# The passage from attention to the first expert layer: where the first expert is counted, when the exponential runs, and where the turned w2 lies

## The chip, the cores and the metric

One core of a Trainium2 chip runs one program. The metric is the device time of one execution in microseconds (us), as the median of several runs. A second number comes from one profiled execution: its span from the first to the last instruction, with every instruction's start and length.

## The reference

```python
scores = scale * np.matmul(z, z.transpose(0, 2, 1))       # 4 batches of 2496 rows, d_qk 64
x = u * np.matmul(np.maximum(scores, 0.0) ** 2, v)        # 9984 rows of 256
# first expert layer, 8 experts, hidden width 1024
do_compute = x @ w_skip > 0
e_idx = argmax(x @ w_gate); gate_w = softmax of the chosen expert
y = gate_w * (relu(x @ w1[e]) @ w2[e]);  x = x + y where do_compute
# second expert layer: logits = x @ w_gate2 + modality_bias[modality_id], the same form, all rows
```

Products are taken in fp32 split into a high and a low part (H and L in the names), three matmuls for one.

## The kernel before

Attention is worked off in 20 chunks of 512 tokens. In each chunk TensorE (PE) makes scores (L1406) and the sums with v (L1417), ScalarE (ACT) takes relu and square, VectorE (DVE) splits the result into AH and AL. One chunk behind, each chunk's 512 rows are routed: PE makes the logits (`route`, L1476) and turns the rows (L1465 in `transpose_x`), DVE picks the experts (`pick_experts`, L1003 to L1019), ACT takes the exponential (`exp_chunk`, L662) and copies the rows (`xrow_half`, L658), PE counts the ranks (`prefixes`, L1488), DVE sets gates (`set_gates`, L1032) and addresses (`place_rows`, L1048 to L1052), and GpSimd (POOL) scatters the rows into `token_rows` in HBM, one indirect DMA for each 128 rows (`scatter_chunk`, L522). Each group of rows (expert of layer one, or of layer two for rows that skip layer one) has its own stretch of `token_rows`, and `base` counts them.

After the last chunk there is no attention work left beside the routing; this stretch is called the passage below. Each engine has its own queue and does its instructions in the order in which its block is written; they meet at semaphores.

- PE: 48 filling matmuls (`keep_warm`), `route`, 6 fillers, `route_rows`, 34 fillers, `prefixes`, `gate_columns(0)` (L1535), `transpose_in` of the first tile (L1553), 16 fillers, the wait for `cum_ready`, then for each expert `gate_parts` (L1545), `gate_columns` of the next expert, and the expert's tiles of 256 rows.
- DVE: sums and product with u, `row_meta` (L991, waits for the scatter of the chunk before), counting of the first expert (`plan_first`), `pick_experts`, `set_gates`, `place_rows`, `finish_groups` (the tile bounds `cum`, last instruction L1187, which sets `cum_ready`), `xt_low`, `plan_second`, a wait for the last scatter, the low part of the gate columns (L1279), the tiles.
- ACT: `sums`, `xrow_half` 0 and 1, `copy_gcols(0)` (L747), `exp_chunk`, the first tile's copies (L777, L778), the wait for `cum_ready`, then for each expert `gpart_split_high` and `copy_gcols` of the next.
- POOL: scatter of chunk 19, `load_w2t(0)` (L483, 1 MB), a wait for `gate_columns(0)`, `load_w2t(1)` into the same place, scatter of chunk 20 (L522; numbers count routed chunks from 1).
- SP: waits for `early_ready` (from `plan_first`) and for the scatter of chunk 19, then loads the first expert's full tiles (L378).

Gate columns are w2 of an expert times the second layer's gate weights; with them the tile's own second product also gives the next layer's logits. `gate_columns(e)` needs w2 of expert e with its axes turned (`w2t_raw`), and lies in the buffer A, which is attention's.

A tile of layer one is 24 matmuls (`layer1(0)`, L1604), four turns, 24 matmuls (`layer1(2)`) and 48 of `layer2` (L1621). The first `layer2` needs the first low part from DVE (`h_low(0)`, L1285). Before its first tile DVE waits on all scattered rows:

```python
xt_low(0, 0)
plan_second()
dve.wait_ge(rows_stored, 64 * (CHUNKS + 1))
```

Of the kernel before, what the change touches and what calls it, by code (L numbers as in the profile page):

```python
# [15 lines left out]
P = 128  # L16
# [44 lines left out]
def bass_attention_two_moe(nc, u, v, z, w_skip, w_gate, w1, w2, modality, w_gate2, bias2, w2t, out):  # L61
    xs = nc.dram_tensor("token_rows", (GR * CAP + SPARE, ROW), F32, kind="Internal").ap()

    with ExitStack() as ctx:
# [6 lines left out]
        def sem(name):  # L71
            return ctx.enter_context(nc.semaphore(name))
# [50 lines left out]
        R = [sb(f"R{i}", [P, QW]) for i in range(2)]  # L123
        A_all = sb("A", [P, NA * QW])
        A = [A_all[:, i * QW:(i + 1) * QW] for i in range(NA)]
        w2t_raw = A_all[:, 0:KD * F].rearrange("p (k f) -> p k f", k=KD)
# [108 lines left out]
        w2t_loaded = sem("w2t_loaded")  # L235
# [208 lines left out]
        def _(pool):  # L444
# [36 lines left out]
            def load_w2t(e):  # L481

                pool.dma_start(w2t_raw, w2t[e, :, :].rearrange("(k p) f -> p k f", p=P)).then_inc(w2t_loaded, 16)  # L483
# [85 lines left out]
            scatter_chunk(CHUNKS - 1)  # L569
            wait(al_ready, 2 + KT * CHUNKS)  # L570
            load_w2t(0)
            wait(gcols_made, 1)
# [10 lines left out]
            for ph in range(2):  # L583
# [14 lines left out]
                for at in range(E):  # L598
# [3 lines left out]
                    def ahead():  # L602
                        if ph == 0:
                            if at + 2 < E:
                                wait(gcols_made, at + 2)
                                load_w2t(at + 2)
                            next_weights(turn_, at % 2, False)
                        else:
                            with pool.If(hi < total):
                                next_weights(turn_, at % 2, True)  # L610
# [26 lines left out]
        def _(act):  # L637
# [120 lines left out]
            xrow_half(CHUNKS, 0)  # L758
            xrow_half(CHUNKS, 1)
            copy_gcols(0)  # L760
            exp_chunk(CHUNKS)

            for ph in range(1):
# [14 lines left out]
                s_.copy(xkeep[:, 0:1, :, :].rearrange("p o s d -> p (o s d)"), xin[:, :, :].rearrange("p s d -> p (s d)")).then_inc(q.x_kept, 1)  # L778
                act.wait_ge(cum_ready, ph + 1)
# [15 lines left out]
                for at in range(E):  # L795
                    hi = end_of(act, ph, at)
                    turn_, h = at + ph * E, at % 2
                    if ph == 0:
                        gpart_split_high(at)
                        if at + 1 < E:  # L800
                            copy_gcols(at + 1)
# [130 lines left out]
        def _(dve):  # L932
# [145 lines left out]
            V_AT = {0: (1,), 1: (2, 3), 2: (4,), 5: (5, 6), 6: (7,), 7: (8,), 8: (9,)}  # L1078
            z_low(0)
# [27 lines left out]
            final_done = [0]  # L1107

            def f(ins):

                final_done[0] += 1
                ins.then_inc(final_step, 1)
                dve.wait_ge(final_step, final_done[0])

            def by_turn(out_, in_):
                f(v_.tensor_tensor(pair[:, 0:E, :], perm[:, :, :], in_[:, None, :].to_broadcast([P, E, E]), ALU.mult))
                f(v_.tensor_reduce(out_, pair[:, 0:E, :], AX.X, ALU.add))

            def full_first(ph, rows):

                f(v_.tensor_scalar(early_f[:, ph:ph + 1], rows, float(TILE[ph]), None, ALU.is_ge))
                f(v_.tensor_scalar(two_f[:, :], rows, float(2 * TILE[ph]), None, ALU.is_ge))
                f(v_.tensor_tensor(early_f[:, ph:ph + 1], early_f[:, ph:ph + 1], two_f[:, :], ALU.add))
                v_.tensor_copy(early[:, ph:ph + 1], early_f[:, ph:ph + 1]).then_inc(early_ready, 1)

# [21 lines left out]
            def plan_first(ph):  # L1150

                full_first(ph, cnt[:, 0:1])

            dve.wait_ge(u_loaded, 16 * CHUNKS)
            for d in range(KD):
                sum_rows(CHUNKS, d).then_inc(o_summed, 1)
                dve.wait_ge(o_summed, 2 * CHUNKS + 1 + d)
                v_.tensor_tensor(xT[:, d, :], xT[:, d, :], uT[:, d, :], ALU.mult).then_inc(x_ready, 1)
            row_meta(CHUNKS)

            dve.wait_ge(base_ready, CHUNKS)
            f(v_.tensor_tensor(cnt[:, :], base[:, :], group0[:, :], ALU.subtract))
            plan_first(0)
            pick_experts(CHUNKS)
# [39 lines left out]
            for ph in range(1):  # L1204
# [61 lines left out]

                xt_low(0, 0)
                if ph == 0:
                    plan_second()
                    dve.wait_ge(rows_stored, 64 * (CHUNKS + 1))  # L1270
                lo = 0
                for at in range(E):
                    hi = end_of(dve, ph, at)
                    turn_ = at + ph * E
                    if ph == 0:
                        dve.wait_ge(gpart_high, at + 1)
                        for s in range(2):
                            part, wh, wl = gate_part(s, at % 2)
                            ins = v_.tensor_tensor(wl, part, wh.bitcast(F32), ALU.subtract)  # L1279
                        ins.then_inc(gpart_low, 1)  # L1280
# [102 lines left out]
        def _(pe):  # L1383
# [142 lines left out]
            def gate_columns(e):  # L1526

                pe.wait_ge(w2t_loaded, 16 * e + 16)
                if e > 0:
                    pe.wait_ge(gcols_copied, e)  # L1530
                for q in range(2):
                    for kd in range(KD):
                        for j in range(QT):
                            f = q * QT + j
                            last = t_.matmul(pO[CG * j:CG * j + CG, 2 * QW + q * P:2 * QW + (q + 1) * P], wg[:, kd, :], w2t_raw[:, kd, f * P:(f + 1) * P],  # L1535
                                             start=(kd == 0), stop=(kd == KD - 1), skip_group_check=True)
# [19 lines left out]
            keep_warm(pS[0], 48)  # L1556
# [3 lines left out]
            keep_warm(pS[0], 34)  # L1560
            prefixes(CHUNKS)
            gate_columns(0)
            pe.wait_ge(xrow_copied, 2 * CHUNKS + 2)

            for ph in range(1):
# [3 lines left out]
                keep_warm(pS[0], 16)  # L1569
# [10 lines left out]
                for at in range(E):  # L1580
                    hi = end_of(pe, ph, at)
                    h = at % 2
                    if ph == 0:
# [177 lines left out]
```

## Time and profile before

| what | us |
|---|---|
| median of 3 runs (lowest to highest) | 1518.81 (1516.99 to 1521.19) |
| the profiled execution's own time | 1520.95 |
| its span | 1519.4 |
| PE busy | 1480.8 (97%) |
| DVE, ACT, POOL busy | 1010.5, 772.6, 398.6 |
| the last attention matmul starts | 725.7 |
| the first expert matmul starts | 744.23 |

Times in rows are from the span's start. A row of a timeline is a run of like instructions on one engine; in brackets stands how long the engine had been idle and who released it. A name such as `pO<-A,wg` is the tile written and those read. The granted clock is PE's, as a share of 2.4 GHz. The end of a matmul is modelled, so starts are the safer reading.

### The profile page before, as it was taken

The page shows a single profiled execution, that of the slowest core. Times are in us where ns is not written, and L with a number is a line of the kernel's source. Part 1 is how long each engine was busy: PE and PEld are TensorE (multiplying, and loading weights), DVE is VectorE, ACT ScalarE, POOL GpSimd, SP SyncE. Part 2 cuts the span into 40 slices and gives each one's busy share as a digit, 9 for nine tenths or more (in the row PEclk, how much of TensorE's full clock was granted, in tenths as well). Part 3 has the DMA queues.
Part 4 walks back from the last instruction along what each step waited for, and adds up shares of the span by engine and source line. Part 5 has one row for each costly group of instructions (what it writes and reads, how often), then busy time and mean ns, then how long its engine had stood idle before and what let it go on. Part 6 is the DMA issues. An engine that isn't in the chain of part 4 may idle for free.

```text
span 1519.4 us, 34233 instructions
## 1 busy us (share of the span) xinstructions
PE 1480.8 (97%) x11713; PEld 1285.9 (85%) x11713; DVE 1010.5 (67%) x2377; ACT 772.6 (51%) x1504; POOL 398.6 (26%) x371
## 2 busy tenths in 40 slices
PE   8999999999999999999899999999999999999995
PEld 7887888788887888788799999998888888888884
DVE  7989987999779998977566666665333433333331
ACT  6676766776666767666344444444332333333331
POOL 4133312334223433311222232224221221211211
PEclk9999999999999999999999999999999999999998
DMA  5302030202312020200433363322211121111110
GB/s 118 98 30 64 28 99 28 65 30 58 90 32 68 28 83 30 85 30 28 162 101 132 131 217 131 105 95 83 86 54 43 42 68 45 42 50 50 42 47 24
DMA packets 57888, 107.83 MB, mean 71 GB/s; under 512 B 17879, under 2 KB 32226, under 8 KB 57756
## 3 DMA queue, kind: packets, MB, share of 16 engines
q0 software_dynamic: 18336, 58.68, 11.0%
q1 hardware_dynamic: 39420, 47.48, 11.0%
q8 instruction: 72, 1.18, 0.3%
q14 instruction: 60, 0.49, 0.1%
HBM read 75.63 MB, written 32.04 MB: 71 GB/s over the span
## 4 chain that ended last, share of the span: by engine, by line
PE 85%; DVE 5%; issue 4%; DMA 3%; POOL 1%; ACT 1%; SPq 0%; POOLq 0%; ACTq 0%; DVEq 0%
PE pO L1417 26%; PE pS L1661 11%; PE pO L1673 10%; PE pS L1621 9%; PE pO L1604 9%; PE pS L1406 7%; PE pO L1675 5%; PE pM L1661 3%; DVE AH L1073 2%; DMA raw<-in_v_dram 2%; PE pT L1652 1%; PE pT L1465 1%; DMA token_rows<-xrow,dest 1%; DVE AL L1075 1%; PE pT L1553 1%
## 5 line engine op out<-in xcount | busy, mean ns | idle before, releaser
L1075 DVE TENSOR_TENSOR AL<-A,AH 128x512 fp32r<-128x512 f32 (+1 forms) x400 | 318.4, 796 | 13.7
L1417 PE MATMUL pO<-AH,VH 64*128 64x512 f32 (+1 forms) x1520 | 299.5, 384 | 6.6 <-DVE xT L983 4.8
L1417 PE MATMUL pO<-AL,VH 64*128 64x512 f32 (+1 forms) x1520 | 298.0, 382 | 0.0
L1417 PE MATMUL pO<-AH,VL 64*128 64x512 f32 (+1 forms) x1520 | 297.8, 381 | 0.0
L695 ACT ACTIVATE R<-pS 128x512 f32<-128x512 f32 (+1 forms) x400 | 213.7, 588 | 149.5 <-PE pS L1406 141.1
L1073 DVE CAST AH<-A 128x512 fp32r<-128x512 f32 (+1 forms) x400 | 222.7, 557 | 42.4 <-ACT A L704 41.8
L704 ACT ACTIVATE A<-R 128x512 f32<-128x512 f32 (+1 forms) x400 | 228.8, 624 | 15.9 <-DVE AL L1075 15.7
L1673 PE MATMUL pO<-VL,AH 128*128 128x512 f32 x640 | 232.4, 399 | 0.0
L1332 DVE SCALAR_TENSOR_TENSOR AL<-pS,AH 128x512 fp32r<-128x512 f32 x120 | 83.0, 692 | 180.1 <-ACT AH L861 179.3
L1675 PE MATMUL pO<-VL,AL 128*128 128x256 f32 x640 | 179.5, 280 | 0.0
L1417 PEld LDWEIGHTS pO<-AH,VH 64*128 64x128 f32 x1520 | 147.8, 184 | 33.6 <-issue 9.2
L580 POOL DMA_INDIRECT out_dram<-xrow,tok_at x80 | 77.9, 974 | 368.2 <-DVE xrow L1342 349.9
L861 ACT ACTIVATE AH<-pS 128x512 fp32r<-128x512 f32 x120 | 71.8, 599 | 195.2 <-PE pS L1661 193.0
L1417 PEld LDWEIGHTS pO<-AL,VH 64*128 64x128 f32 x1520 | 147.8, 184 | 23.0
L1417 PEld LDWEIGHTS pO<-AH,VL 64*128 64x128 f32 x1520 | 147.9, 184 | 22.4
L1661 PE MATMUL pS<-ZH,VH 128*128 (+1 forms) x480 | 165.1, 391 | 0.7 <-issue 0.4
L1673 PEld LDWEIGHTS pO<-VL,AH 128*128 128x128 f32 x640 | 120.2, 188 | 25.6
L1604 PE MATMUL pO<-ZH,VH 128*128 x736 | 129.6, 289 | 0.0
L541 POOL TENSOR_TENSOR xT<-xT,uT 128x512 f32<-128x512 f32 x38 | 50.5, 1340 | 300.6 <-DVE xT L983 300.6
L1675 PEld LDWEIGHTS pO<-VL,AL 128*128 128x128 f32 x640 | 120.6, 188 | 3.2
L1621 PE MATMUL pS<-VL,AH 128*128 128x264 f32 x736 | 120.7, 286 | 0.0
L522 POOL DMA_INDIRECT token_rows<-xrow,dest x80 | 85.9, 1074 | 101.0 <-issue 99.8
(232 smaller groups left out, 2412.3 us busy)
## 6 DMA issues: line engine op xcount, KB each, us to landing
raw<-in_w_dram POOLq DMA_DIRECT2D x22, 1024.0 KB
A<-token_rows SPq DMA_DIRECT2D x21, 536.0 KB
uT<-in_u_dram SPq DMA_DIRECT2D x16, 512.0 KB
A<-in_w2t_dram POOLq DMA_DIRECT2D x8, 1024.0 KB
xin<-token_rows SPq DMA_DIRECT2D x24, 268.0 KB
raw<-in_v_dram SPq DMA_DIRECT2D x4, 1152.0 KB, 6.0
raw<-in_v_dram SPq DMA_DIRECT2D x4, 768.0 KB, 7.7
raw<-in_z_dram SPq DMA_DIRECT2D x8, 368.0 KB
```

Of the source, the lines that this page charges most:

```text
L522: g_.indirect_dma_start(xs, bass.IndirectOffsetOnAxis(dest[:, j:j + 1], 0), xrow[:, j, :], None, bounds_check=GR * CAP - 1, oob_is_err=Fal ...
L695: s_.activation(R[k % 2][:, 0:n], pS[k % 2][:, 0:n], ACT.Relu, scale=1.0 / S).then_inc(relu_done, 1)
L704: s_.activation(A[k % NA][:, 0:n], R[k % 2][:, 0:n], ACT.Square).then_inc(square_done, 1)
L1073: v_.tensor_copy(AH[k % NBUF][:, 0:n], A[k % NA][:, 0:n]).then_inc(ah_ready, 1)
L1075: v_.tensor_tensor(AL[k % NBUF][:, 0:n], A[k % NA][:, 0:n], AH[k % NBUF][:, 0:n].bitcast(F32), ALU.subtract).then_inc(al_ready, 1)
L1406: last = t_.matmul(pS[r][:, 0:n], w[rows, (2 * p + r) * P:(2 * p + r + 1) * P], x[rows, zc:zc + n], start=(m == 0), stop=(m == 2))
L1417: last = t_.matmul(pO[:, (KD * r + d) * QW:(KD * r + d) * QW + n], vv[rows, vo + k * D + d * P:vo + k * D + (d + 1) * P], a[k % NBUF][rows ...
L1604: last = t_.matmul(pO[:, bank * 512 + fi * TT:bank * 512 + (fi + 1) * TT], w[h][:, kd, f * P:(f + 1) * P], x[:, ds(par, 1), kd, :].rearran ...
L1621: last = t_.matmul(pS[s][:, 0:width], a[p][:, fi * TT + s * P:fi * TT + (s + 1) * P], w[h][:, f, 0:width], start=(f == 0 and n == 0), stop ...
L1661: last = t_.matmul(ring[f % RING][:, :], w[h][:, kd, f * P:(f + 1) * P], x[:, ds(par, 1), kd, :].rearrange("p o t -> p (o t)"), start=(n = ...
L1673: t_.matmul(pO[:, s * QW:(s + 1) * QW].rearrange("p (m d) -> p m d", m=2), AH[f][:, rows], w2hl[h][:, :, f, 0:D], start=(f == 0), stop=(f ...
L1675: last = t_.matmul(pO[:, s * QW:s * QW + D], AL[f][:, rows], w2h[h][:, f, 0:D], start=False, stop=(f == NF - 1), skip_group_check=True)
```

## The change

- DVE counts the first expert (`plan_first`) inside the last attention chunk, after `place_rows(19)`. After the sums it goes straight to `pick_experts`; `row_meta` comes behind that.
- ACT takes the exponential between the two halves of `xrow_half`. `gpart_split_high(0)` and `copy_gcols(1)` come ahead of the wait for `cum_ready`.
- The turned w2 has two places: A for even experts, and for odd ones the unused end of `raw` together with R (two buffers made one). Each load is two DMAs of 512 KB. `load_w2t(0)` comes ahead of the scatter of chunk 19, `load_w2t(1)` behind it and behind the last attention matmul; later loads wait for one `gate_columns` less.
- DVE makes the low part of expert 0's gate columns ahead of `plan_second` and of the wait for the scattered rows.
- PE: 40 fillers ahead of `route` in place of 48; `gate_columns(0)` and 6 fillers ahead of `prefixes` in place of 34 fillers; `gate_parts(0)`, `gate_columns(1)` and 40 fillers ahead of the wait for `cum_ready`, in place of 16 fillers there and of the two gate steps behind it.

```diff
-        R = [sb(f"R{i}", [P, QW]) for i in range(2)]
+        R_all = sb("R", [P, 2 * QW])
+        R = [R_all[:, i * QW:(i + 1) * QW] for i in range(2)]
-        w2t_raw = A_all[:, 0:KD * F].rearrange("p (k f) -> p k f", k=KD)
+        w2t_raw = [[A_all[:, 0:F], A_all[:, F:2 * F]], [raw[:, 2 * KD * F:(2 * KD + 1) * F], R_all[:, :]]]
...
@@ POOL
-                pool.dma_start(w2t_raw, w2t[e, :, :].rearrange("(k p) f -> p k f", p=P)).then_inc(w2t_loaded, 16)
+                for kd in range(KD):
+                    pool.dma_start(w2t_raw[e % 2][kd], w2t[e, kd * P:(kd + 1) * P, :]).then_inc(w2t_loaded[e % 2], 16)
...
-            scatter_chunk(CHUNKS - 1)
             wait(al_ready, 2 + KT * CHUNKS)
             load_w2t(0)
-            wait(gcols_made, 1)
+            scatter_chunk(CHUNKS - 1)
+            wait(pv_done, NBUF + KT * CHUNKS)
             load_w2t(1)
             scatter_chunk(CHUNKS)
...
-                                wait(gcols_made, at + 2)
+                                wait(gcols_made, at + 1)
                                 load_w2t(at + 2)
@@ ACT
             xrow_half(CHUNKS, 0)
+            exp_chunk(CHUNKS)
             xrow_half(CHUNKS, 1)
             copy_gcols(0)
-            exp_chunk(CHUNKS)
...
+                gpart_split_high(0)
+                copy_gcols(1)
                 act.wait_ge(cum_ready, ph + 1)
...
-                    if ph == 0:
+                    if at > 0:
                         gpart_split_high(at)
@@ DVE
                             place_rows(g)
+                            dve.wait_ge(base_ready, CHUNKS)
+                            plan_first(0)
...
+            pick_experts(CHUNKS)
             row_meta(CHUNKS)
-
-            dve.wait_ge(base_ready, CHUNKS)
-            f(v_.tensor_tensor(cnt[:, :], base[:, :], group0[:, :], ALU.subtract))
-            plan_first(0)
-            pick_experts(CHUNKS)
             set_gates(CHUNKS)
             place_rows(CHUNKS)
...
                 xt_low(0, 0)
+                gate_low(0)
                 if ph == 0:
                     plan_second()
@@ PE
-                pe.wait_ge(w2t_loaded, 16 * e + 16)
+                pe.wait_ge(w2t_loaded[e % 2], 32 * (e // 2) + 32)
...
-            keep_warm(pS[0], 48)
+            keep_warm(pS[0], 40)
             route(CHUNKS)
             keep_warm(pS[0], 6)
             route_rows(CHUNKS)
-            keep_warm(pS[0], 34)
+            gate_columns(0)
+            keep_warm(pS[0], 6)
             prefixes(CHUNKS)
-            gate_columns(0)
             pe.wait_ge(xrow_copied, 2 * CHUNKS + 2)
...
                 transpose_in(q, 0)
-                keep_warm(pS[0], 16)
+                gate_parts(0)
+                gate_columns(1)
+                keep_warm(pS[0], 40)
                 pe.wait_ge(cum_ready, ph + 1)
...
-                    if ph == 0:
+                    if at > 0:
                         gate_parts(at)
```

The functions `f`, `by_turn`, `full_first` and `plan_first` of DVE move up in the text so that they can be called earlier, and the low part of the gate columns becomes a function `gate_low`; what they issue is the same.

## Rows read from the trace of the kernel before

**Rows 1.** The page: engine, busy us (share of the span), instructions.

```profile
PE 1480.8 (97%) x11713; PEld 1285.9 (85%) x11713; DVE 1010.5 (67%) x2377; ACT 772.6 (51%) x1504; POOL 398.6 (26%) x371
```

**Rows 2.** Chain of waits, 660 to 800 us: start, length, what took it.

```profile
729.03 6.26 DMA A<-in_w2t_dram
...
736.85 0.16 ACT ex L662
...
740.50 0.18 DVE pad_from L1187
740.68 0.89 issue
```

**Rows 3.** Timeline of PE, 712 to 752 us: start, length, operation, [idle before, releaser].

```profile
726.03 2.85 PE L1393 MATMUL pS<-ones 128*128 128x128 bf16 x48
...
729.42 0.66 PE L1476 MATMUL pM<-xT,wg 128*32 128x128 f32 x13 [0.20 <-issue]
...
731.37 0.66 PE L1465 MATMUL pT<-ident,xT 128*128 128x128 f32 x4 [0.36 <-ACT xrow L658]
...
734.10 0.21 PE L1488 MATMUL pM<-oh,before 128*128 128x80 bf16 x1 [0.18 <-DVE oh L1019]
...
741.56 0.69 PE L1545 MATMUL pO<-ident,gcols 128*128 128x128 f32 x2 [3.67 <-DVE pad_from L1187]
742.36 1.94 PE L1535 MATMUL pO<-A,wg 128*32 128x128 f32 x32
744.23 0.80 PE L1604 MATMUL pO<-ZH,VH 128*128 x2
```

**Rows 4.** Timeline of PE, 748 to 786 us.

```profile
752.23 0.65 PE L1621 MATMUL pS<-VL,AH 128*128 128x264 f32 x4
...
758.04 0.40 PE L1604 MATMUL pO<-ZH,VH 128*128 x2
...
764.23 0.65 PE L1621 MATMUL pS<-VL,AH 128*128 128x264 f32 x4
...
782.73 1.08 PE L1535 MATMUL pO<-A,wg 128*32 128x128 f32 x32
```

**Rows 5.** Timeline of DVE, 712 to 752 us.

```profile
725.01 0.69 DVE L983 TENSOR_TENSOR xT<-pO,xT 128x512 f32<-128x512 f32 x1 [2.30 <-ACT xT L652]
...
727.49 0.69 DVE L1158 TENSOR_TENSOR xT<-xT,uT 128x512 f32<-128x512 f32 x1
730.67 0.17 DVE L991 COPY xrow<-meta 128x12 f32<-128x12 f32 x1 [2.50 <-DMA token_rows<-xrow,dest]
...
731.60 0.31 DVE L1003 STREAM_TRANSPOSE logits<-pM 128x128 f32<-128x128 f32 x1
...
733.82 0.23 DVE L1019 TENSOR_TENSOR oh<-eq,take 128x64 bf16<-128x64 f32 x1
...
738.02 0.22 DVE L1048 TENSOR_TENSOR rank<-pM,base 128x64 f32<-128x64 f32 x1
...
747.56 0.29 DVE L1279 TENSOR_TENSOR VL<-pO,VL 128x32 fp32r<-128x32 f32 x2 [1.84 <-DMA token_rows<-xrow,dest]
```

**Rows 6.** Timeline of POOL, 690 to 830 us.

```profile
723.78 0.97 POOL L522 DMA_INDIRECT token_rows<-xrow,dest  x1 [15.83 <-issue]
...
737.06 0.75 POOL L483 DMA_DIRECT2D A<-in_w2t_dram  x1 [7.28 <-PE pO L1535]
...
744.09 0.97 POOL L522 DMA_INDIRECT token_rows<-xrow,dest  x1 [0.30 <-issue]
```

**Rows 7.** Timeline of SP's queue, 690 to 830 us.

```profile
732.98 5.77 SPq L378 DMA_DIRECT2D xin<-token_rows  x2
```

**Rows 8.** Stretches: length, engines' busy time, granted clock, DMA share, GB/s.

```profile
741.00:741.50 0.50, 0.00 (x0) 0.00 (x0) 0.50 (x2) 0.00 (x0) 0.20 (x2) 0.82 1.05 434
744.00:747.50 3.50, 3.50 (x23) 3.28 (x16) 1.51 (x9) 0.37 (x1) 0.97 (x1) 0.50 0.41 140
```

**Rows 9.** Waits of PE from 744 us to the end: us in total, times, longest.

```profile
PE pS L1661 <- issue: 0.4, 1, 0.4
```

More of the change, by code:

```diff
@@ L234, in bass_attention_two_moe @@
         wl_ready = sem("wl_ready")
-        w2t_loaded = sem("w2t_loaded")
+        w2t_loaded = [sem(f"w2t_loaded{i}") for i in range(2)]
         gcols_made = sem("gcols_made")
@@ L1078, in _, with f, by_turn, full_first @@
             V_AT = {0: (1,), 1: (2, 3), 2: (4,), 5: (5, 6), 6: (7,), 7: (8,), 8: (9,)}
+            final_done = [0]
+            def f(ins):
+                final_done[0] += 1
+                ins.then_inc(final_step, 1)
+                dve.wait_ge(final_step, final_done[0])
+            def by_turn(out_, in_):
+                f(v_.tensor_tensor(pair[:, 0:E, :], perm[:, :, :], in_[:, None, :].to_broadcast([P, E, E]), ALU.mult))
+                f(v_.tensor_reduce(out_, pair[:, 0:E, :], AX.X, ALU.add))
+            def full_first(ph, rows):
+                f(v_.tensor_scalar(early_f[:, ph:ph + 1], rows, float(TILE[ph]), None, ALU.is_ge))
+                f(v_.tensor_scalar(two_f[:, :], rows, float(2 * TILE[ph]), None, ALU.is_ge))
+                f(v_.tensor_tensor(early_f[:, ph:ph + 1], early_f[:, ph:ph + 1], two_f[:, :], ALU.add))
+                v_.tensor_copy(early[:, ph:ph + 1], early_f[:, ph:ph + 1]).then_inc(early_ready, 1)
+            def plan_first(ph):
+                f(v_.tensor_tensor(cnt[:, :], base[:, :], group0[:, :], ALU.subtract))
+                full_first(ph, cnt[:, 0:1])
             z_low(0)
@@ L1106, in _ @@
                             place_rows(g)
[L1107 to L1124, printed above, removed]
+                            dve.wait_ge(base_ready, CHUNKS)
+                            plan_first(0)
             def plan_counts():
@@ L1148, in plan_order @@
                 v_.tensor_copy(order[:, :], order_f[:, :])
-            def plan_first(ph):
-                full_first(ph, cnt[:, 0:1])
             dve.wait_ge(u_loaded, 16 * CHUNKS)
@@ L1265, in next_low, with gate_low @@
                         v_.tensor_tensor(wl, raw, wh.bitcast(F32), ALU.subtract).then_inc(wl_ready, 1)
+                def gate_low(e):
+                    dve.wait_ge(gpart_high, e + 1)
+                    for s in range(2):
+                        part, wh, wl = gate_part(s, e % 2)
+                        ins = v_.tensor_tensor(wl, part, wh.bitcast(F32), ALU.subtract)
+                    ins.then_inc(gpart_low, 1)
                 xt_low(0, 0)
+                gate_low(0)
                 if ph == 0:
@@ L1274, in _ @@
                     turn_ = at + ph * E
-                    if ph == 0:
[L1276 to L1280, printed above, removed]
+                    if at > 0:
+                        gate_low(at)
                     with dve.If(lo < hi):
@@ L1534, in gate_columns @@
                             f = q * QT + j
-                            last = t_.matmul(pO[CG * j:CG * j + CG, 2 * QW + q * P:2 * QW + (q + 1) * P], wg[:, kd, :], w2t_raw[:, kd, f * P:(f + 1) * P],
+                            last = t_.matmul(pO[CG * j:CG * j + CG, 2 * QW + q * P:2 * QW + (q + 1) * P], wg[:, kd, :], w2t_raw[e % 2][kd][:, f * P:(f + 1) * P],
                                              start=(kd == 0), stop=(kd == KD - 1), skip_group_check=True)
@@ L1582, in _ @@
                     h = at % 2
-                    if ph == 0:
+                    if at > 0:
                         gate_parts(at)
```

## The prediction

> **What bounds the kernel now.** I read the page first: PE is busy for 97% of the span [rows 1], so away from the few places where PE waits, nothing that another engine does can move the end. PE's waits from 744 us to the end have 0.4 us as the longest [rows 9]: once the first expert tile runs, the whole rest follows it at a fixed distance. The attention part is not touched. So the question is by how much the first expert matmul starts earlier, and how fast the tile behind it runs.
>
> Second, the timeline of PE in the passage. The last attention matmul is out by 726.03 us and the first expert matmul starts at 744.23 us [rows 3]. In these 18.2 us PE does fillers and a few short steps. Third, the chain of waits there: a landing of the turned w2 at 735.29 us, gate columns, the exponential (which stands behind them in ACT's order), gates and addresses, tile bounds ready at 740.68 us, and 0.89 us more until PE's next matmul [rows 2]. Fourth, the stretches. PE stood idle 3.67 us before 741.56 us [rows 3]. In that idle time the granted clock fell: 0.82 over 741.0 to 741.5 us and 0.50 over 744.0 to 747.5 us [rows 8], that is the lower level, 1.2 GHz, in place of 2.4 GHz. The first tile pays for it: from its first matmul (744.23) to its first second-layer matmul (752.23) are 8.00 us, in the next tile (758.04 to 764.23) 6.19 us [rows 3, 4]. The gate columns of expert 1 took 1.94 us at that clock, those of expert 2 1.08 us [rows 3, 4].
>
> **The change part by part.**
>
> *Eight fillers fewer.* 48 take 2.85 us, 0.059 us each [rows 3]. x is complete at 727.49 + 0.69 = 728.2 us [rows 5], and 40 fillers end at 728.4 us. So the route product ends at 729.42 + 0.66 - 0.47 = 729.6 us.
>
> *Picking without waiting.* Before, DVE waited 2.5 us for the scatter of chunk 19 and then counted the first expert; picking began at 731.60 us and ended at 734.05 us [rows 5]. After, it begins at 729.6 us and ends at about 732.05 us. The counting moves to the 2.30 us in which DVE waits for ACT ahead of 725.01 us [rows 5]; it is as long as the stretch from 730.67 to 731.60 us at most, 0.93 us, so it costs nothing. Without that cover it would delay x by up to 0.9 us.
>
> *Turned w2 of expert 0 ahead of the scatter.* Its two calls on POOL take 0.75 us each by the row of one call [rows 6]. POOL had been idle for 15.83 us before the scatter of chunk 19 began at 723.78 us [rows 6], and the load only needs the last split on DVE, which in DVE's order comes before the addresses for which the scatter waits. Bounds of the delay of the scatter: 0 (both calls lie in the idle time) and 1.5 us (both behind it). I take 0.3 us, near the lower end, since the addresses take DVE about 1 us more after the split. What stands behind the scatter is ACT's first row copy, SP's load of the first tile, DVE's `row_meta`, and POOL's next load. The scatter was seen by DVE at 730.67 us [rows 5]; after, 731.0 us.
>
> *PE up to the ranks.* The second row turns began at 731.37 us, released by ACT's first copy [rows 3]; after, 731.7 us. With 0.5 us of turns (the row's 0.66 us less the overlap of its modelled end), 1.08 us for `gate_columns(0)` [rows 4], 6 fillers (0.35 us) and 0.4 us for the five small matmuls of the ranks (the first is 0.21 us [rows 3], the others overlap it; an estimate), these are ready at 734.0 us. The exponential now runs on ACT right behind the first copy, at about 731.7 us, in place of 736.85 us [rows 2], and the gates are done before the ranks.
>
> *Bounds of the tiles.* From `place_rows` (738.02 us) to the last bound (740.68 us) are 2.66 us [rows 2, 5]. After: 734.0 + 2.7 = 736.7 us, 4.0 us earlier. This alone is no longer the end of the chain.
>
> *What is late next: expert 1's gate columns and 40 fillers.* `load_w2t(1)` is called when the scatter's calls are through: 729.03 us before [rows 2], 729.3 us now. One load of 1 MB took 6.26 us [rows 2]; expert 1's took no more than 742.36 - 737.06 = 5.30 us [rows 3, 6]. Two halves land between 734.6 us (5.30 us for both) and 736.4 us (6.26 us, counted from a second call 0.75 us later). The tile of x, loaded at 732.98 us [rows 7] and now some 0.7 us earlier because the count is ready long before, was turned right after gate columns that began at 735.3 us, so it lands by 735.7 us, and with 0.9 us of turns and gate turns PE is at the gate columns by 736.6 us at the latest. I take 736.0 us, inside both. Then 1.08 us and 40 fillers, 2.4 us: 739.5 us. Entering the loop cost 0.89 us when nothing was queued [rows 2]; behind fillers it may cost nothing. Between 0 and 0.9 us I take 0.3 us, as expert 2's gate steps at 782.73 us follow a tile without such a gap [rows 4]. First expert matmul: 739.8 us in place of 744.23 us, 4.4 us.
>
> A rule that speaks against the two halves: by the Trainium skill, "DMA: Bandwidth & Descriptors", section "Anatomy of one DMA", a DMA costs about 2 us plus its bytes at 436 GB/s, so a whole megabyte 4.4 us and two halves 6.4 us if they don't overlap. By that the gate columns would begin near 735.7 us, within my bounds; the row of 6.26 us for one undivided load is already longer than the rule.
>
> *The clock.* PE's longest idle stretch is now about 1.5 us (ranks to x, then to w2), far below the 3.67 us in whose course it fell, and 2.4 us of fillers come straight before the tile. So the first tile runs at 2.4 GHz: 8.00 - 6.19 = 1.8 us.
>
> *Without cost.* The earlier `gate_low`, `gpart_split_high(0)` and `copy_gcols(1)`: they lie under the 2.4 us of fillers. Eight more DMA calls of 0.75 us on POOL, which is busy 26% [rows 1]; without that cover they would delay weight loads, which PE doesn't wait for now [rows 9]. The wait for all scattered rows on DVE: before, it ended by 747.56 us [rows 5], 3.5 us after POOL's last call at 744.09 us [rows 6]. The addresses come 4.0 us earlier, so it ends at 743.5 us. The tile's second product starts at 739.8 + 6.2 = 746.0 us and needs 0.7 us of DVE first: 1.8 us to spare, 0.9 us of loop entry included or not.
>
> **Sum.** 4.4 + 1.8 = 6.2 us. The profiled execution took 1520.95 us by itself with a span of 1519.4 us; it would take 1514.75 us and 1513.2 us. It lies 2.1 us above the median of the runs, within their scatter, so the median goes from 1518.8 to 1512.6 us (0.41%). The case's own bounds: 736.6 and 0.9 us give 741.0 us, a gain of 5.0 us; 734.6 and 0 give 738.1 us, a gain of 7.9 us. That is 1510.9 to 1513.8 us.
>
> **The rivals.**
>
> *Something else is late in the first tile.* The halves, the scatter and x share the DMA engines, and two more delays (the scatter by its full 1.5 us, w2 as much behind it) would start the tile at 741.5 us; or DVE meets the scattered rows too late and the second product waits. For it: each step hangs on landings. Against: the slack of 1.8 us. Gain 3.5 to 5 us, about 1514.6 us. Chance 0.17.
>
> *The clock falls all the same.* PE does little between 733 and 737 us. Then gate columns cost 0.9 us more, the fillers 2.4 us more, and the tile keeps its 1.8 us: gain 6.2 - 5.1 = 1.1 us, 1517.7 us. Against: before, it fell only in the longest idle stretch of the passage, 3.67 us [rows 3]. Chance 0.10.
>
> *Slower.* POOL's loads now stand ahead of both last scatters. If the calls of the scatter and of `load_w2t(1)` had to wait until expert 0's w2 had landed, that load would land late. The point that decides is about 739.7 us: PE would then have been idle over 3.3 us and at 1.2 GHz; gate columns 1.94 us and fillers 4.8 us lead to 746.4 us, 2.2 us later than before, 1521.0 us. Against: the calls of a scatter were followed by w2's call without a gap. Chance 0.05.
>
> **How the numbers follow.** The forecast has 0.68. A measurement of this kernel can tell about 0.3%, 4.6 us, from no change. The forecast's case lies beyond that but for its slow end and the scatter of medians (0.65 of 0.68), and the first rival in part (0.05): faster 0.70. Within: 0.25. Slower 0.05. The range of 1510.3 to 1516.6 us takes in the forecast's bounds with 0.6 us of scatter and the first rival, and leaves out the clock case and the slower one, 0.15.
>
> **What the profile after would show.** Picking (L1003's line) at 729.6 us; the exponential near 731.7 us; bounds ready at 736.7 us; gate columns of expert 1 near 736.0 us, 1.1 us long; granted clock 1.00 throughout; first L1604-line matmul at 739.8 us and its tile 6.2 us to the second product. It would be wrong if w2 of expert 1 or x lands after 737 us, if the clock falls before the fillers, or if PE waits inside the first tile.

## The result, and the profile after

The changed kernel took 1514.76 us (median of 8 runs, 1513.94 to 1518.43), the kernel before 1518.89 us (8 runs beside them, 1516.99 to 1521.19). The ratio is 0.9968, with a 95% interval of 0.9959 to 0.9977: faster by 0.23 to 0.41%. The medians differ by 4.1 us. The ratio stands for 4.9 us of 1518.89 (its interval for 3.5 to 6.2 us), and a second comparison, after2 below, gave 5.0 us. Forecast were 6.2 us.

The profiled execution of after took 1518.43 us with a span of 1516.9 us, 3.7 us above its median. Attention, which is unchanged, ended 1.72 us later in it than in the profile before (first filler at 727.75 us against 726.03 us [rows 3]), because the granted clock had fallen once at 303 to 307 us, after an idle stretch of 1.51 us (the last section has the rows). So times in the passage are compared from the end of attention, that is from the first filler.

The timeline of PE in the passage, after (start, length, operation, [idle before, releaser]):

```profile
727.75 2.41 PE L1398 MATMUL pS<-ones 128*128 128x128 bf16 x40
...
733.04 0.66 PE L1470 MATMUL pT<-ident,xT 128*128 128x128 f32 x4 [1.39 <-ACT xrow L660]
733.62 1.08 PE L1540 MATMUL pO<-A,wg 128*32 128x128 f32 x32
...
734.98 0.20 PE L1493 MATMUL pM<-oh,before 128*128 128x80 bf16 x1
...
737.01 0.66 PE L1558 MATMUL pT<-ident,xin 128*128 128x128 f32 x4 [1.74 <-DMA xin<-token_rows]
737.50 0.38 PE L1550 MATMUL pO<-ident,gcols 128*128 128x128 f32 x2
737.81 0.42 PE L1540 MATMUL pO<-raw,wg 128*32 128x128 f32 x8
...
738.83 2.41 PE L1398 MATMUL pS<-ones 128*128 128x128 bf16 x40
742.15 0.50 PE L1611 MATMUL pO<-ZH,VH 128*128 x2 [0.92 <-issue]
...
748.44 0.65 PE L1628 MATMUL pS<-VL,AH 128*128 128x264 f32 x4
```

The first expert matmul (L1611) comes 14.40 us after attention, against 744.23 - 726.03 = 18.20 us [rows 3]: 3.8 us gained. From there to the second product (L1628) are 6.29 us, against 8.00 us: 1.7 us more. The longest idle stretch is 1.74 us and no longer 3.67 us. It ends when x lands; what used to end it, the bounds on DVE, is ready at 737.95 us, while PE is still at the gate columns.

The timeline of DVE in the same stretch:

```profile
730.80 0.32 DVE L1007 STREAM_TRANSPOSE logits<-pM 128x128 f32<-128x128 f32 x1 [0.91 <-PE pM L1481]
733.02 0.22 DVE L1023 TENSOR_TENSOR oh<-eq,take 128x64 bf16<-128x64 f32 x1
...
735.30 0.23 DVE L1052 TENSOR_TENSOR rank<-pM,base 128x64 f32<-128x64 f32 x1 [0.92 <-PE pM L1495]
...
737.79 0.16 DVE L1187 CAST pad_from<-base 128x8 int32<-128x8 f32 x1
```

The timeline of ACT:

```profile
732.40 0.58 ACT L660 COPY xrow<-pT 128x512 f32<-128x512 f32 x1 [3.96 <-DMA token_rows<-xrow,dest]
732.88 0.26 ACT L664 ACTIVATE ex<-lsh 128x64 f32<-128x64 f32 x1
```

The timeline of POOL, where expert 0's two halves are called ahead of the scatter and expert 1's second half at 731.31 us:

```profile
723.62 1.17 POOL L485 DMA_DIRECT2D A<-in_w2t_dram  x2 [13.98 <-DVE AL L1079]
...
731.31 0.58 POOL L485 DMA_DIRECT2D R<-in_w2t_dram  x1
```

Picking waits for the logits alone and starts 3.05 us after attention (before, 731.60 - 726.03 = 5.57 us [rows 5]). The exponential runs at 732.88 us behind ACT's first copy, and not behind the gate columns [rows 2].

The stretches over the passage (length, busy time of PE, its weight loads, DVE, ACT, POOL, then the granted clock, DMA share, GB/s) show the upper level, 2.4 GHz, throughout, where [rows 8] had 0.82 and 0.50:

```profile
733.00:736.00 3.00, 2.23 (x47) 1.77 (x47) 1.85 (x12) 1.09 (x3) 0.00 (x0) 1.00 0.93 353
736.00:739.00 3.00, 1.99 (x41) 1.63 (x42) 2.32 (x12) 1.30 (x5) 1.28 (x2) 1.00 0.12 41
...
742.00:745.00 3.00, 2.85 (x23) 2.85 (x24) 1.68 (x10) 0.00 (x0) 0.28 (x1) 1.00 0.43 152
```

At the second product after is 5.5 us ahead (20.69 us after attention against 26.20), at the end of the span only 4.2 us (789.15 against 793.37). The 1.3 us between are given back behind the passage. PE's waits from 744 us to the end (us in total, times, longest) were three before, of which [rows 9] has the longest. The other two:

```profile
PE pT L1652 <- issue: 0.3, 1, 0.3
PE pS L1661 <- DVE ZL L1326: 0.3, 1, 0.3
```

After:

```profile
PE pT L1659 <- DMA A<-token_rows: 0.5, 1, 0.5
PE pT L1659 <- issue: 0.4, 1, 0.4
PE pO L1659 <- DMA A<-token_rows: 0.3, 1, 0.3
PE pS L1668 <- issue: 0.3, 1, 0.3
PE pS L1668 <- DVE ZL L1331: 0.3, 1, 0.3
```

These sum to 1.8 us, against 1.0 us before, and lie in the second expert layer; two of the five rows name the landing of a tile's rows. Second traces of the two kernels have 1.7 us and 1.5 us, so at most a part of the 1.3 us lies in these waits. From the second product to the row `pO<-ident,A`, at the start of the second layer, both traces of after took 283.4 us, those of before 282.9 and 283.1 us. From there to the end the second trace of after took 0.1 us less than before, and this one 0.8 us more. So the cost behind the passage differs between executions: it is 1.3 us here and 0.4 us in the second trace.

### The profile page after: what moved, and what is told of

Its sections match the earlier page's. It is cut to its first block, busy times and chain, and to the rows that moved or that the text cites. A ratio compares the mean times of both kernels' runs of the same rounds, so it can differ in the third digit from the quotient of the medians.

```text
span 1516.9 us, 34217 instructions
## 1 busy us (share of the span) xinstructions
PE 1477.9 (97%) x11701; PEld 1284.2 (85%) x11701; DVE 1010.0 (67%) x2377; ACT 771.3 (51%) x1504; POOL 401.0 (26%) x379
## 4 chain that ended last, share of the span: by engine, by line
PE 82%; DVE 5%; issue 5%; DMA 4%; ACT 1%; POOL 1%; SPq 1%; POOLq 0%; ACTq 0%; DVEq 0%
PE pO L1422 24%; PE pS L1668 11%; PE pO L1680 10%; PE pO L1611 9%; PE pS L1628 9%; PE pS L1411 6%; PE pO L1682 5%; PE pM L1668 3%; DVE AH L1077 3%; DMA raw<-in_v_dram 2%; PE pT L1659 1%; DMA token_rows<-xrow,dest 1%; PE pT L1470 1%; DVE AL L1079 1%; DMA A<-token_rows 1%
## 5 line engine op out<-in xcount | busy, mean ns | idle before, releaser
L1611 PE MATMUL pO<-ZH,VH 128*128 x736 | 128.3, 286 | 1.0 <-issue 0.9
L1628 PE MATMUL pS<-VL,AH 128*128 128x264 f32 x736 | 120.8, 286 | 0.0
L824 ACT ACTIVATE AH<-pO 128x512 fp32r<-128x512 f32 x92 | 52.6, 597 | 118.5 <-PE pO L1611 118.5
```

Of the source, the lines that this page charges most:

```text
L1611: last = t_.matmul(pO[:, bank * 512 + fi * TT:bank * 512 + (fi + 1) * TT], w[h][:, kd, f * P:(f + 1) * P], x[:, ds(par, 1), kd, :].rearran ...
L1628: last = t_.matmul(pS[s][:, 0:width], a[p][:, fi * TT + s * P:fi * TT + (s + 1) * P], w[h][:, f, 0:width], start=(f == 0 and n == 0), stop ...
```

## The experiments

The question was where one to two of the six forecast microseconds had gone, and which part carries the rest. The first theory: the 40 fillers and the loop's entry behind them now stand on the path, and the clock doesn't need them. Its rival: the fillers hold the clock, and without them the tile pays. For the gain itself: either the clock by itself is worth its 1.8 us, or it is worth nothing while something else holds the tile. Each kernel ran beside the kernel before on the same chip. Rows with the same time for before shared a chip, and kernels from different chips are compared by their ratios. The last two columns are from one trace each, us after the end of attention.

| kernel | median us | before, same chip | ratio (95%) | first expert matmul | second product |
|---|---|---|---|---|---|
| before | 1518.89 | | | 18.20 | 26.20 |
| after | 1514.76 | 1518.89 | 0.9968 (0.9959 to 0.9977) | 14.40 | 20.69 |
| a_fill0 | 1512.60 | 1519.69 | 0.9953 (0.9940 to 0.9967) | 12.05 | 18.80 |
| a_fill16 | 1514.17 | 1519.69 | 0.9962 (0.9948 to 0.9975) | 12.93 | 19.21 |
| a_exp_late | 1513.83 | 1519.69 | 0.9961 (0.9948 to 0.9975) | 14.19 | 20.47 |
| b_fill60 | 1520.11 | 1519.69 | 1.0005 (0.9996 to 1.0014) | 16.80 | 24.47 |
| after2 | 1514.09 | 1519.08 | 0.9967 (0.9955 to 0.9979) | 14.08 | 20.36 |
| a_fill0_rows | 1512.49 | 1519.08 | 0.9956 (0.9942 to 0.9970) | 12.01 | 18.29 |
| b_fill60_gate | 1518.92 | 1519.08 | 0.9998 (0.9988 to 1.0007) | 17.33 | 24.47 |
| a_w2t_late | 1519.05 | 1519.08 | 1.0002 (0.9993 to 1.0011) | 17.69 | 23.97 |
| b_again | 1521.73 | 1521.17 | 0.9999 (0.9989 to 1.0009) | 18.46 | 26.48 |
| a_wide11 | 1516.81 | 1521.17 | 0.9971 (0.9960 to 0.9982) | 13.27 | 21.15 |
| a_best | 1515.56 | 1521.17 | 0.9966 (0.9953 to 0.9978) | 12.02 | 19.96 |
| a_dve_old | 1522.84 | 1521.17 | 1.0006 (0.9997 to 1.0015) | 19.12 | 26.83 |

**after2 and b_again: the two kernels once more.** No edit.

> The changed kernel itself once more, so that the others of this call have it on the same chip. 4.1 to 5.5 us below the kernel before; first expert matmul 14.4 us after the end of attention, second product of the first tile 20.7 us after it.

> The kernel before itself once more, for a second trace of it on this chip: how far the stretches outside the passage vary between executions. Passage as before: first expert matmul 18.2 us after the end of attention, second product 26.2 us after it, granted clock 0.50 around the first tile. From the second product to the end of the span 767.2 us in the first trace; if that varies by over 1 us, it explains why the runs with fillers in the kernel before had 1.4 us less in their traces and nothing less in their medians. Ratio 1.000.

Both came out as they had: 0.9967 beside 0.9968 for after, 0.9999 for before against itself. The marks in the passage move by 0.3 us from one trace of a kernel to the next. From the second product to the end before took 767.2 and 767.3 us, after 768.5 and 767.5 us. So what b_again was to look for, a scatter of over 1 us there in the kernel before, was not seen.

**a_fill0 and a_fill16: fewer fillers ahead of the first tile.**

```diff
                 gate_columns(1)
-                keep_warm(pS[0], 40)
+                keep_warm(pS[0], 16)      # a_fill16; a_fill0 has no such line
                 pe.wait_ge(cum_ready, ph + 1)
```

> The changed kernel without the 40 fillers ahead of the wait for the tile bounds. Theory 1, the fillers lie on the path and nothing needs them: gate columns of expert 1 end at 738.8 us after attention that ends at 727.75 us, the bounds are ready at 737.95 us, so the first expert matmul starts near 738.9 us in place of 742.15 us (11.2 us after the end of attention in place of 14.4 us), granted clock 1.00 throughout; about 1511.6 us, or up to 0.5 us more if DVE meets the scattered rows too late. Rival, the fillers hold the clock: it falls to 0.50 around the first tile, the tile takes up to 8 us in place of 6.3 us, and the time is 1513 to 1515 us.

> The changed kernel with 16 fillers in place of 40 at the same place. Theory 1: 24 fillers fewer are 1.4 us, first expert matmul 13.0 us after the end of attention, about 1513.4 us. Rival: 16 are too few, the clock falls in the first tile and nothing or less than 0.5 us is won, 1514.3 us or more. If the run without fillers keeps its clock, this one must too.

PE's timeline in a_fill0, and one of its stretches (columns as above):

```profile
734.94 0.40 PE L1540 MATMUL pO<-R,wg 128*32 128x128 f32 x8
736.37 0.49 PE L1610 MATMUL pO<-ZH,VH 128*128 x2 [1.03 <-DVE ZL L1215]
...
743.12 0.75 PE L1627 MATMUL pS<-VL,AH 128*128 128x264 f32 x4 [0.30 <-DVE AL L1290]
```

```profile
736.00:739.00 3.00, 2.63 (x22) 2.63 (x23) 2.59 (x14) 0.00 (x0) 2.39 (x3) 1.00 0.62 189
```

The clock stays up without them, so the rival falls. The tile starts 2.35 us earlier than in after, and the median gains about 2 us: by the ratios, 0.9953 and 0.9968, it is 2.3 us, but from two chips and with intervals that overlap. Beside after2 on one chip, a_fill0_rows below gains 1.6 us, with no run above 1513.26 us, where after2's are 1513.18 us and more. Not all of fillers and entry, 3.3 us, is won: behind the last gate columns PE stands 1.03 us. The row names the low part of x, but DVE's timeline has that ready at 735.53 us, 0.84 us before the tile, and the bounds at 734.64 us; the loop's entry isn't hidden behind the gate columns either. And inside the tile a new wait of 0.30 us appears: the low part of the first hidden block began only when the scattered rows had landed. a_fill16 lies between the two in its trace and in its ratio.

**a_fill0_rows: that wait moved behind the tile's work.** a_fill0, and

```diff
                     plan_second()
-                    dve.wait_ge(rows_stored, 64 * (CHUNKS + 1))
...
                             dve.wait_ge(q.h_used, 4 * t + 8)
+                            dve.wait_ge(rows_stored, 64 * (CHUNKS + 1))
```

> The changed kernel without the 40 fillers, and DVE's wait for all scattered rows moved from ahead of the tiles to just ahead of the first write into the rows' buffer at a tile's end. Theory 1: without the fillers PE waited 0.3 us for the first low part, which DVE made 1.2 us after the rows had landed; now that part follows ACT, the second product starts 18.2 us after the end of attention in place of 18.8 us, and the time is 0.5 us below that of the run without fillers, about 2.5 us below the changed kernel on this chip. Rival: the wait on DVE costs nothing, same time as without fillers.

The second product comes 6.28 us after the first expert matmul and no longer 6.75 us; the median is that of a_fill0. Among PE's waits from 743 us on, one for a tile's rows in the second layer is 1.2 us long, more than the half microsecond won:

```profile
PE pT L1658 <- DMA A<-token_rows: 1.2, 1, 1.2
```

**b_fill60: the kernel before with its clock held up.** Does the clock by itself bring 1.8 us?

```diff
                 transpose_in(q, 0)
-                keep_warm(pS[0], 16)
+                keep_warm(pS[0], 60)
                 pe.wait_ge(cum_ready, ph + 1)
```

> The kernel before with 60 fillers in place of 16 ahead of its wait for the tile bounds; they end at about 740.4 us, before the bounds at 740.7 us. This is the clock's part of the gain alone. Theory 1: granted clock 1.00, gate columns of expert 1 in 1.08 us in place of 1.94 us, first tile in 6.2 us in place of 8.0 us to its second product: 2.7 us less, about 1516.2 us. Rival, the low clock in the first tile is not due to the idle 3.67 us: still 0.50 there, 1518.9 us.

The timeline of PE, then DVE's, in b_fill60:

```profile
742.14 1.08 PE L1535 MATMUL pO<-A,wg 128*32 128x128 f32 x32 [0.48 <-DMA A<-in_w2t_dram]
...
747.94 0.48 PE L1604 MATMUL pO<-ZH,VH 128*128 x2 [1.15 <-DVE VL L1279]
...
750.89 0.29 PE L1621 MATMUL pS<-VL,AH 128*128 128x264 f32 x1
```

```profile
747.51 0.29 DVE L1279 TENSOR_TENSOR VL<-pO,VL 128x32 fp32r<-128x32 f32 x2 [2.11 <-DMA token_rows<-xrow,dest]
```

The clock is held: the gate columns take 1.08 us, not 1.94 [rows 3], and the mean granted clock of its executions is 0.994 or 0.995, against 0.993 or 0.994 for before on that chip. The median gains nothing, though in the trace the first tile begins 1.4 us earlier and the second product comes 1.7 us earlier. The tile is fast for its first half, then PE stands for the low part of the gate columns, which DVE makes behind the wait for the last scattered rows. That landing comes 21.1 us after attention here, and in before 21.5 us [rows 5], at either clock. So of the tile's 1.8 us only 0.3 are left (7.67 us to the second product against 8.00), and the tile needs the earlier addresses to have the rest. In after the last call of the scatter on POOL begins 13.6 us after attention, before 18.1 us. Why the 1.7 us at the second product don't show in the median stays open.

**b_fill60_gate: the low part ahead of that wait.** b_fill60, and

```diff
                 xt_low(0, 0)
+                gate_low(0)
                 if ph == 0:
                     plan_second()
```

> The kernel before with 60 fillers in place of 16 ahead of its wait for the tile bounds, and the low part of expert 0's gate columns ahead of the plan of the second layer and of the wait for the scattered rows. Theory 1: the clock alone won little because at full clock the tile's second half waited 1.15 us for that low part; with both, the second product starts 23.0 us after the end of attention (26.2 us before, 24.5 us with fillers alone), 3.2 us less time than before. Rival: a tile that starts earlier gives its gain back later, as the run with fillers alone measured no gain at all: within 1 us of before.

The chain of waits in b_fill60_gate:

```profile
742.85 4.64 DMA token_rows<-xrow,dest
...
748.69 0.70 DVE AL L1290
...
749.43 2.68 PE pS L1626 x20
```

The 23.0 us expected for the second product were missed: it comes at 24.47 us as in b_fill60. The first half of the tile no longer waits, but the next thing behind the same landing does, the first hidden block's low part. The rows land at 747.49 us, 22.5 us after attention, and from there DVE takes 1.2 us to enter its own loop. The second product comes 1.94 us behind that landing; had the rows landed at 21.1 us as in b_fill60, that would have been the 23.0 us expected. So the floor of these tiles is the landing and not the order of `gate_low`, and it came 1.4 us later here. The median shows no gain.

**a_w2t_late: the turned w2 of expert 0 behind the scatter again.**

```diff
-            load_w2t(0)
             scatter_chunk(CHUNKS - 1)
+            load_w2t(0)
```

> The changed kernel with the load of expert 0's turned w2 behind the scatter of chunk 19 again (both places and the rest kept). Theory 1: that load lands 9 us after the end of attention, gate columns 0 stand ahead of the ranks and delay them by 3 us, bounds ready at 13 us, and the first expert matmul starts about 15.9 us after the end of attention in place of 14.4 us: 1.5 us more than the changed kernel. Rival: the load's place in POOL's order is without effect, no change.

The timeline of PE and a stretch:

```profile
734.36 1.93 PE L1540 MATMUL pO<-A,wg 128*32 128x128 f32 x32 [3.37 <-DMA A<-in_w2t_dram]
...
736.84 0.27 PE L1493 MATMUL pM<-oh,before 128*128 128x80 bf16 x1
```

```profile
734.00:736.00 2.00, 1.64 (x32) 1.38 (x32) 0.00 (x0) 0.00 (x0) 0.00 (x0) 0.58 1.03 413
```

This one line takes the whole gain in the median. PE waits 3.37 us for w2, the clock falls to its lower level (0.58 over 734 to 736 us), the gate columns take 1.93 us, and the ranks, which stand behind them in PE's order, come 4.5 us later than in after (11.73 us after attention against 7.23). In its one trace the second product is 2.2 us and the end 1.5 us earlier than in that of before; its median does not show this. The trace is not typical here: its execution had a mean granted clock of 0.994, and nine of the other ten had 0.992 or 0.993, at or below the 0.993 or 0.994 of before on that chip. So in most of them the clock was low for longer; 0.001 to 0.002 of 1517 us are 1.5 to 3 us, by an estimate from these rounded numbers.

**a_exp_late: the exponential behind the copies again.**

```diff
             xrow_half(CHUNKS, 0)
-            exp_chunk(CHUNKS)
             xrow_half(CHUNKS, 1)
             copy_gcols(0)
+            exp_chunk(CHUNKS)
```

> The changed kernel with the exponential back behind both row copies and the copy of the gate columns on ACT. Theory 1, this part buys nothing as long as PE has gate columns and 40 fillers to do: bounds ready about 1 us later (near 739 us), still ahead of the fillers' end at 741.2 us; 1514.8 us, no change against the changed kernel. Rival, the exponential's place is a large part of the gain: 1 to 3 us more, 1516 to 1518 us.

The timeline of PE:

```profile
730.88 0.74 PE L1470 MATMUL pT<-ident,xT 128*128 128x128 f32 x4 [1.76 <-ACT xrow L660]
731.55 1.94 PE L1540 MATMUL pO<-A,wg 128*32 128x128 f32 x32
```

Nothing is lost (0.9961 beside 0.9967 and 0.9968). The bounds are ready 12.5 us after attention and not 10.2 us, but the fillers end only at 13.6 us. So with 2.4 us of fillers ahead of the tile the exponential's place doesn't matter. Whether it does without the fillers was not tried; a_fill0's tile starts at 12.05 us, ahead of these bounds. The same trace shows the clock fall inside the changed passage: behind an idle stretch of 1.76 us expert 0's gate columns take 1.94 us and not 1.08. Over 736 to 738 us, under the fillers, it was back at 1.00.

**a_dve_old: DVE's order as before.**

```diff
-                            dve.wait_ge(base_ready, CHUNKS)
-                            plan_first(0)
...
-            pick_experts(CHUNKS)
             row_meta(CHUNKS)
+            dve.wait_ge(base_ready, CHUNKS)
+            plan_first(0)
+            pick_experts(CHUNKS)
             set_gates(CHUNKS)
```

> The changed kernel with DVE's old order behind the last sums: the copy into the rows that waits for the scatter of chunk 19, then the count of the first expert, then the picking. Theory 1: the bounds come 1.4 us later, which the fillers hide, but the count sets the load of the first tile 0.9 us later, and with it everything that PE does behind it: first expert matmul 15.3 us after the end of attention in place of 14.4 us, 0.9 us more time than the changed kernel. Rival: this order is the largest part of the gain, 2.5 us more time.

The timeline of PE:

```profile
738.31 1.07 PE L1398 MATMUL pS<-ones 128*128 128x128 bf16 x16
739.81 0.27 PE L1398 MATMUL pS<-ones 128*128 128x128 bf16 x2 [0.43 <-issue]
740.59 0.22 PE L1398 MATMUL pS<-ones 128*128 128x128 bf16 x1 [0.50 <-issue]
...
743.52 2.08 PE L1398 MATMUL pS<-ones 128*128 128x128 bf16 x18 [1.14 <-issue]
745.52 0.79 PE L1611 MATMUL pO<-ZH,VH 128*128 x2
```

The expectation was missed by far. Up to the gate columns of expert 1 the passage is 0.8 us behind after (10.90 us after attention against 10.06), as expected. Then PE, which has nothing to wait for among its fillers, gets its instructions in drops, with five gaps of 0.43 to 1.14 us, 3.1 us in all; the granted clock falls to 0.50, and the tile starts at 19.12 us. PE's program is the same as in after. All of its eleven runs lie between 1520.35 and 1523.31 us, so the lost time is no chance of one trace; that the gaps are the same in each of them is not shown. After was not run on this chip. Beside a_wide11, which was, a_dve_old loses 6.0 us.

**a_wide11: the same filling time in 11 matmuls of 512 columns.**

```diff
-                keep_warm(pS[0], 40)
+                for _ in range(11):
+                    t_.matmul(pS[0][:, :].rearrange("p (a b) -> p a b", a=4), ones[:, :],
+                              ones[:, None, :].to_broadcast([P, 4, P]), start=True, stop=True)
```

> The changed kernel with 11 fillers of 512 columns in place of 40 of 128 ahead of the wait for the tile bounds: as long on PE (2.4 us), a quarter of the instructions. Theory 1: PE's queue of instructions couldn't get ahead of 58 ns fillers, so entering the loop cost 0.92 us behind them; behind 0.22 us fillers it can, the 0.92 us vanish, the first expert matmul starts 13.4 us after the end of attention in place of 14.4 us, 0.9 us less time. Rival: the entry never overlaps what PE does ahead of it, start at 14.3 us, no change.

The timeline of PE:

```profile
738.37 2.55 PE L1577 MATMUL pS<-ones 128*128 128x512 bf16 x11
740.56 0.59 PE L1612 MATMUL pO<-ZH,VH 128*128 x2
...
741.41 0.42 PE L1612 MATMUL pO<-ZH,VH 128*128 x2
742.90 0.47 PE L1612 MATMUL pO<-ZH,VH 128*128 x2 [1.07 <-issue]
```

The entry is hidden, as expected: no gap ahead of the tile, which starts at 13.27 us. But a gap of 1.07 us without a releaser stands inside it, and the tile takes 7.88 us to the second product, so in the trace more is lost inside it than the hidden entry won. The ratio is that of after.

**a_best: a_fill0_rows with the ranks ahead of the gate columns.**

```diff
-            gate_columns(0)
-            keep_warm(pS[0], 6)
             prefixes(CHUNKS)
+            gate_columns(0)
```

> The changed kernel without the 40 fillers, with DVE's wait for the scattered rows at the first tile's end, and with the ranks ahead of the gate columns of expert 0 and without the 6 fillers between. Theory 1: the ranks waited 1.7 us for gate columns and fillers while DVE stood idle 0.9 us; now the bounds come 0.9 us earlier, the first expert matmul starts 11.2 us after the end of attention (12.0 us without this), the second product 17.4 us after it; 0.8 us less than the run without fillers, about 3 us less than the changed kernel. Rival: x of the first tile, whose load waits for the scatter, is the bound already at 12.0 us: no gain over the run without fillers.

It isn't better. The ranks are counted 0.8 us earlier than in a_fill0, but the bounds come only 0.1 us earlier (10.2 us), as DVE still has the gates to do, and x lands no earlier (9.3 us against 9.1). So the first tile starts where that of a_fill0_rows does (12.02 us), 0.7 us after the low part of x is ready, and three gaps of 0.18 to 0.47 us without a releaser lie in it. The fastest kernels of the study are a_fill0 and a_fill0_rows, which can't be told apart: 1512.6 and 1512.5 us, 0.9953 and 0.9956 of before.

## Why the prediction was right, and where it was not

The direction, the range (1510.3 to 1516.6 us) and the cause held; the gain is two thirds of the 6.2 us by the medians, four fifths by the ratios. The forecast's own bounds, 1510.9 to 1513.8 us, were missed by 1 us by the median: the range held because it took in the first rival. That rival's number, about 1514.6 us, is nearly the measured one, but its mechanism did not come. No load came late, the tile started 14.40 us after attention where the rival needs 15.5, and PE waited for nothing inside it. So that agreement is luck. Times are after the end of attention.

- **The scatter of chunk 19** was to slip 0.3 us behind the load of w2. ACT, which waits for its landing, goes on at 4.65 us; before, DVE went on from it at 4.64 us [rows 3, 5]: no slip. Both calls lay in POOL's idle time.
- **Picking** was to start at 3.6 us and started at 3.05. The ranks reached DVE at 7.55 us; forecast were 8.0. The bounds are ready at 10.2 us; forecast were 10.7.
- **The gate columns of expert 1** were to begin at 10.0 us and began at 10.06. The halves of w2 were not what was waited for, x was. Their issues in after (size, us from the call to the landing):

```profile
raw<-in_w2t_dram POOLq DMA_DIRECT2D x1, 512.0 KB, 4.3
R<-in_w2t_dram POOLq DMA_DIRECT2D x1, 512.0 KB, 5.0
```

  The calls began at 730.73 and 731.31 us, so the halves landed at about 735.0 and 736.3 us, 1.3 us apart and 5.6 us after the first call: they were loaded largely at once. By the Trainium skill ("DMA: Bandwidth & Descriptors", section "Anatomy of one DMA") a DMA costs about 2 us plus its bytes at 436 GB/s, an estimate of 3.2 us for one half and 6.4 us for two one behind the other. The trace doesn't bear out the 6.4 us, which would be 737.1 us; each half by itself took longer than 3.2 us.

- **The term that was mis-sized is "Entering the loop cost 0.89 us when nothing was queued [rows 2]; behind fillers it may cost nothing. Between 0 and 0.9 us I take 0.3 us".** It cost 0.92 us, as though nothing were queued (0.71 in a second trace, 0.64 and 0.86 in a_exp_late and a_w2t_late, 0.70 behind 16 fillers). That is the whole difference between the forecast 13.8 us and the 14.40 us of this trace, and 0.6 of the 2.0 us by which the trace falls short of 6.2 us at the end of the span. a_wide11 shows the other end: behind 11 long fillers no gap stands ahead of the tile.
- **The fillers** were counted rightly, 2.4 us, but the step took them as given. a_fill0 and a_fill0_rows show that they aren't needed to hold the clock and cost about 2 us.
- **The clock** term of 1.8 us measured 1.7. What the prediction put under "without cost", the earlier rows and the earlier `gate_low`, is what makes it real in the tile: b_fill60 has the clock without these and wins 0.3 us of it there. The ground on which the clock was trusted, idle stretches "far below the 3.67 us", was weak: after stood idle for 1.74 us in the passage and kept 1.00, a_exp_late stood 1.76 us and fell to 0.50. That it held had luck in it.
- **"The whole rest follows it at a fixed distance"** holds only roughly: 5.5 us at the second product are 4.2 us at the end of the span, 1.3 us less and the largest part of the shortfall in this trace. In the second trace 5.8 us become 5.5 us. PE's waits in the second layer, 1.0 us in all before, are 1.8 and 1.7 us.

Of the rivals, the one that ended slower did not come: the loads took no time from the scatters. The one in which the clock falls came in a_w2t_late and a_dve_old, and there the median gain is gone.

Three things stay open. One trace each of b_fill60 and a_w2t_late ends 1.4 to 1.5 us closer to attention than that of before, and their medians show no gain; for a_w2t_late the granted clocks of the other executions point to the reason, for b_fill60 nothing does. The clock's fall inside attention, 1.6 us in both traces of after, is outside of every sum here; whether executions without a trace had it can't be told. And what holds PE's instructions back in a_dve_old, a_wide11 and a_best is not settled.

## What to carry to other kernels

Work that was put in to bridge a wait stands on the path once the wait is gone: after such a change, take it out again and look at the clock. A gain on one resource shows only when the next landing behind it has moved as well, so look for what the same semaphore holds elsewhere (here the scattered rows). A passage that hands over among five engines is a chain of nearly equal waits; in the medians, undoing one part of it, the load order on POOL or the order on DVE, cost everything that the others had brought, and undoing the exponential's place cost nothing.

## What the hardware did that was not expected

PE can stand 0.4 to 1.1 us, several times in a row, in the midst of matmuls that wait for nothing that the profile shows. In a_dve_old 5 such gaps sum to 3.1 us, in a_wide11 one is 1.07 us, in a_best three sum to 1.1 us. They lie 13 to 17 us after the end of attention, in the stretch in which the last scatter and the first tiles' loads run. After itself has none there but the loop's entry. PE's program is the same in after and a_dve_old, so its code alone is not the reason. The three kernels ran on one chip; b_again, on the same, shows no such gap longer than 0.33 us in the passage, and after was not run there. All four traces from this chip have one more, of 0.32 to 0.34 us, before or in the route product; of the ten other traces only that of before has one there, of 0.20 us. That speaks for the chip as part of it. Whether the chip, the timing or the supply of instructions is behind it was not tested. The profile's two instruction queues moved no packet between 738 and 746 us in a_dve_old, so none of its five gaps ends at one.

The granted clock can fall behind a short idle stretch too: to 0.56 and 0.58 over 303 to 307 us in after, where PE had stood 1.51 us, and in after2 at the same place behind 1.68 us. The same stretches of before show 1.00. The length of the stretch alone doesn't decide: a_fill16 stood 1.95 us and a_w2t_late 1.47 us at the same place, and both kept 1.00. None of the twelve other traces has the fall there, though eight of their programs do the same as after up to that point. It costs 1.6 us: ahead of it after is 0.1 us behind before, past it 1.7 us. After's (columns as above):

```profile
303.00:305.00 2.00, 2.00 (x12) 1.85 (x14) 1.97 (x3) 2.00 (x6) 2.00 (x2) 0.56 0.00 0
305.00:307.00 2.00, 2.00 (x14) 1.85 (x12) 1.97 (x3) 1.11 (x3) 0.67 (x1) 0.58 0.15 22
```
